# Routed tiles of 256 slots instead of 384, and the gather two tiles ahead, in a recurrence-plus-two-MoE kernel

## The reference: what is computed

```python
noisy_logits = x @ w_gate + np.log1p(np.exp(x @ w_noise)) * noise
top2 = np.argpartition(-noisy_logits, 2, axis=1)[:, :2]
...
for e in range(E):                       # E = 8 experts
    for k in range(2):
        mask = top2[:, k] == e
        h = np.maximum(x[mask] @ w1[e], 0.0)          # 384 -> 1024
        out[mask] += top2_w[mask, k, None] * (h @ w2[e])   # 1024 -> 384
```

## Time and profile before

| | |
|---|---|
| time, 3 runs | median 2584.08 us (2580.21 to 2586.68) |
| span of the profiled execution | 2575.4 us; a time of its own beside the span is not on record |
| PE busy | 2442.9 us (95%) |
| DVE, ACT, POOL busy | 1042.4 (40%), 650.6 (25%), 523.1 us (20%) |
| chain that ended last | PE 73%, DMA 8%, issue 6%, DVE 5%, POOL 5% |
| mean granted TensorE clock | 0.981 |

### The profile page before, as it was taken

One profiled execution on the slowest core, in us unless ns is written; L12 is line 12 of the kernel. 1 busy time (PEld: TensorE's weight loads), 2 busy tenths in 40 slices (PEclk: granted clock), 3 DMA queues, 4 the chain that ended last, 5 costly groups with the idle time before them and its releaser, 6 DMA issues.

```text
span 2575.4 us, 40463 instructions
## 1 busy us (share of the span) xinstructions
PE 2442.9 (95%) x14404; PEld 2422.2 (94%) x14404; DVE 1042.4 (40%) x2039; ACT 650.6 (25%) x1165; POOL 523.1 (20%) x327
## 2 busy tenths in 40 slices
PE   7999999999999999999999999999949999999997
PEld 6989999999999999999999999999849998999897
DVE  8992444333333333333333333334533444343433
ACT  3441111111111111111111111114414444444442
POOL 2112101011011011010110110112343333343333
PEclk9999999999999999999999999999969999999999
DMA  5451000000000000000000000003225555455543
GB/s 134 111 163 64 12 13 24 0 25 24 0 24 18 6 24 0 24 24 0 24 24 0 24 24 0 25 0 62 37 70 158 140 157 174 135 142 141 179 143 62
DMA packets 45907, 155.54 MB, mean 60 GB/s; under 512 B 12992, under 2 KB 32320, under 8 KB 37936
## 3 DMA queue, kind: packets, MB, share of 16 engines
q1 hardware_dynamic: 29984, 127.89, 15.4%
q0 software_dynamic: 15888, 27.19, 5.8%
HBM read 130.23 MB, written 24.82 MB: 60 GB/s over the span
## 4 chain that ended last, share of the span: by engine, by line
PE 73%; DMA 8%; issue 6%; DVE 5%; POOL 5%; ACT 1%; another core or an unknown queue 1%; DVEq 0%; ACTq 0%; POOLq 0%; SPq 0%
PE bank L1082 38%; PE bank L1073 31%; DMA xg<-x,slot_in 4%; DMA out_dram<-ys,slot_out 4%; POOL out_dram L417 3%; POOL xg L428 1%; PE bank L1187 1%; DVE inv L648 1%; DVE decay L642 1%; ACT ys L609 1%; PE bank L991 1%; DVE probs L656 1%; PE bank L1129 1%; DVE state L680 0%
## 5 line engine op out<-in xcount | busy, mean ns | idle before, releaser
L1082 PE MATMUL bank<-w_hi,h_hi 128*128 128x384 f32 x2088 | 712.9, 341 | 4.0 <-DVE h_lo L744 4.0
L1082 PE MATMUL bank<-w_lo,h_hi 128*128 128x384 f32 x2088 | 702.8, 337 | 0.0
L1082 PE MATMUL bank<-w_hi,h_lo 128*128 128x384 f32 x2088 | 702.8, 337 | 0.0
L513 ACT ACTIVATE h_hi<-bank 128x384 fp32r<-128x384 f32 x512 | 251.8, 492 | 1343.0 <-PE bank L1073 1313.4
L1073 PE MATMUL bank<-x_hi,w_hi 128*128 (+1 forms) x1536 | 522.1, 340 | 0.0
L1073 PE MATMUL bank<-x_lo,w_hi 128*128 (+1 forms) x1536 | 520.5, 339 | 0.0
L1073 PE MATMUL bank<-x_hi,w_lo 128*128 (+1 forms) x1536 | 520.4, 339 | 0.0
L744 DVE SCALAR_TENSOR_TENSOR h_lo<-bank,h_hi 128x384 fp32r<-128x384 f32 x512 | 284.9, 557 | 392.2 <-ACT h_hi L513 375.4
L755 DVE SCALAR_TENSOR_TENSOR acc<-bank,route,acc 128x384 f32 (+1 forms) x336 | 186.7, 611 | 589.0 <-PE bank L1082 589.0
L1082 PEld LDWEIGHTS bank<-w_hi,h_hi 128*128 128x128 f32 x2088 | 394.5, 189 | 4.6 <-issue 4.6
L1082 PEld LDWEIGHTS bank<-w_lo,h_hi 128*128 128x128 f32 x2088 | 395.0, 189 | 0.0
(11 more groups left out here) (154 smaller groups left out, 1936.9 us busy)
## 6 DMA issues: line engine op xcount, KB each, us to landing
raw<-wts SPq DMA_DIRECT2D x62, 1536.0 KB, 6.5
qka_sb<-qka SPq DMA_DIRECT2D x48, 288.0 KB, 4.7
out_dram<-zrow SPq DMA_DIRECT2D x1, 5376.0 KB, 17.8
v_sb<-v SPq DMA_DIRECT2D x24, 192.0 KB, 2.5
x<-acc SPq DMA_DIRECT2D x8, 576.0 KB
xg<-x,slot_in POOLq DMA_INDIRECT x69, 5.2
out_dram<-ys,slot_out POOLq DMA_INDIRECT x69
x<-zrow SPq DMA_DIRECT2D x1, 768.0 KB, 18.3
```

The source lines that it names most:

```text
L513: act.activation(h_hi[:, f], ps_h[f][:, 0:TW], ACT.Relu).then_inc(s_hh, 1)
L1082: mm = pe.matmul(ps_o[s][:, 0:DM], hx, w, start=(first and n == 0), stop=(last and n == 2))
```

## The change

Tiles hold RW = 256 slots (RS = 2 slices of 128) instead of 384, and there are (2N - E) // 256 + 8 = 31 of them. Up products move 256 columns, h and the token buffers are taken at that width, down products still move 384 columns but for 2 slices. The plan's arithmetic follows (NS = 12 steps of 256). On POOL the first two tiles are fetched ahead of the loop, and in the loop the fetch of tile t+2 comes ahead of the scatter of tile t. The dense stages keep TW = 384.

```diff
+RW = 256
+RS = RW // P
+NS = N // RW
-SLOTS = RI + TW
+SLOTS = RI + RW
-TILES = (2 * N - E) // TW + E
+TILES = (2 * N - E) // RW + E
...
             def prefetch(tile, p):
-                sp.wait_ge(s_gt, SUB * tile + PRIMED)
+                sp.wait_ge(s_gt, RS * tile + PRIMED)
...
             def scatter(tile, p, pair):
-                pool.wait_ge(s_ys, SUB * (tile + 1) + PRIMED)
+                pool.wait_ge(s_ys, RS * (tile + 1) + PRIMED)
-                for s in range(SUB):
+                for s in range(RS):
...
             split_part(2 * E + 1, 1, 1)
-            with pool.Fori(0, TILES // 2) as pair:
+            fetch(1, 1, 0)
+            with pool.Fori(0, (TILES - 2) // 2) as pair:
                 for p in range(2):
-                    fetch(2 * pair + p + 1, 1 - p, pair + p)
+                    fetch(2 * pair + p + 2, p, pair + 1)
                     scatter(2 * pair + p, p, pair)
-            scatter(TILES - 1, (TILES - 1) % 2, (TILES - 1) // 2)
+            fetch(TILES - 1, (TILES - 1) % 2, (TILES - 1) // 2)
+            for tile in range(TILES - 3, TILES):
+                scatter(tile, tile % 2, tile // 2)
...
             def run_step(tile, p, last):                      # scalar
-                        act.activation(h_hi[:, f], ps_h[f][:, 0:TW], ACT.Relu).then_inc(s_rh, 1)
+                        act.activation(h_hi[:, f, 0:RW], ps_h[f][:, 0:RW], ACT.Relu).then_inc(s_rh, 1)
...
-                for s in range(SUB):
+                for s in range(RS):
                     act.activation(ys[:, p, s], ps_o[s][:, 0:DM], ACT.Copy,
...
             def run_step(tile, p, last):                      # tensor
-                        up(f, *w1, lambda k: xg_hi[:, p, k], lambda k: xg_lo[:, p, k]).then_inc(s_ph, 1)
+                        up(f, *w1, lambda k: xg_hi[:, p, k], lambda k: xg_lo[:, p, k], RW).then_inc(s_ph, 1)
...
-                        down(f, *w2, half == 0 and f == 0, half == 1 and f == FC - 1).then_inc(s_dn, 1)
-                        if half == 1 and not last and f < SUB - 1:
+                        down(f, *w2, half == 0 and f == 0, half == 1 and f == FC - 1, RS).then_inc(s_dn, 1)
+                        if half == 1 and not last and f < RS - 1:
                             turn_gathered(tile + 1, 1 - p, f + 1, (tile + 1) // 2)
```

More of the change, by code:

```diff
@@ L135, in recurrence_and_experts @@
         raw2 = sb("raw2", [P, 2, W1C + W2C])
[L136 to L141, removed]
+        slot_in = sb("slot_in", [P, 2, RS, 2])
+        slot_out = sb("slot_out", [P, 2, RS, 2])
+        xg = sb("xg", [P, 2, RS, DM])
+        xg_hi = sb("xg_hi", [P, 2, KD, RW], FP32R)
+        xg_lo = sb("xg_lo", [P, 2, KD, RW], FP32R)
+        ys = sb("ys", [P, 2, RS, DM])
         bank = [pb(f"bank{i}") for i in range(8)]
@@ L285, in load_slots @@
                 sp.dma_start(buffer[:, p].rearrange("p s w -> p (s w)"),
-                             slots[bass.ds(row, TW)].rearrange("(p s) w -> p (s w)", p=P)).then_inc(loaded[p], 16)
+                             slots[bass.ds(row, RW)].rearrange("(p s) w -> p (s w)", p=P)).then_inc(loaded[p], 16)
             def load_unit(expert, half):
@@ L319, in _ @@
             prefetch(TILES - 2, 1)
-            sp.wait_ge(s_add, 16 * SUB * TILES)
+            sp.wait_ge(s_add, 16 * RS * TILES)
             sp.wait_ge(s_x2, 16 * TS)
@@ L583, in take_tokens @@
             def take_tokens(tile, p):
-                for s in range(SUB):
-                    act.wait_ge(s_gt, SUB * tile + s + 1 + PRIMED)
+                for s in range(RS):
+                    act.wait_ge(s_gt, RS * tile + s + 1 + PRIMED)
                     act.activation(xg_hi[:, p, :, s * P:(s + 1) * P],
@@ L890, in _ @@
             steps.link(dve.tensor_copy(count[:, 0], ps_total))
-            steps.link(dve.tensor_tensor(steps_of[:, 1], count[:, 0].unsqueeze(2).to_broadcast([P, E, E]),
+            steps.link(dve.tensor_tensor(steps_of[:, 1], count[:, 0].unsqueeze(2).to_broadcast([P, E, NS]),
                                          steps_of[:, 0], ALU.is_gt))
@@ L920, in low_tokens @@
             def low_tokens(tile, p):
-                for s in range(SUB):
-                    dve.wait_ge(s_gh, SUB * tile + s + 1)
+                for s in range(RS):
+                    dve.wait_ge(s_gh, RS * tile + s + 1)
                     cols = slice(s * P, (s + 1) * P)
@@ L934, in run_step @@
                         dve.wait_ge(s_rh, n * FC + f + 1)
-                        dve.scalar_tensor_tensor(h_lo[:, f], ps_h[f][:, 0:TW], 0.0, h_hi[:, f].bitcast(FP32),
+                        dve.scalar_tensor_tensor(h_lo[:, f, 0:RW], ps_h[f][:, 0:RW], 0.0, h_hi[:, f, 0:RW].bitcast(FP32),
                                                  ALU.max, ALU.subtract).then_inc(s_rl, 1)
@@ L1072, in up, with down @@
                 for n, (w, x) in enumerate(todo):
-                    mm = pe.matmul(ps_h[f][:, 0:TW], w, x, start=(n == 0), stop=(n == len(todo) - 1))
+                    mm = pe.matmul(ps_h[f][:, 0:width], w, x, start=(n == 0), stop=(n == len(todo) - 1))
                 return mm
-            def down(f, w2h, w2l, first, last):
-                for s in range(SUB):
+            def down(f, w2h, w2l, first, last, subs=SUB):
+                for s in range(subs):
                     rows = slice(s * P, (s + 1) * P)
@@ L1182, in turn_gathered @@
             def turn_gathered(tile, p, s, pair):
-                pe.wait_ge(s_gat[p], 16 * SUB * (pair + 1))
+                pe.wait_ge(s_gat[p], 16 * RS * (pair + 1))
                 if gathered_in(tile, s) is ps_xg:
-                    pe.wait_ge(s_gl, SUB * tile + s + PRIMED)
+                    pe.wait_ge(s_gl, RS * tile + s + PRIMED)
                 for k in range(KD):
@@ L1205, in run_step @@
                     if half == 0:
-                        pe.wait_ge(s_ys, SUB * tile + PRIMED)
+                        pe.wait_ge(s_ys, RS * tile + PRIMED)
                     for f in range(FC):
                         pe.wait_ge(s_rl, n * FC + f + 1)
-                        down(f, *w2, half == 0 and f == 0, half == 1 and f == FC - 1).then_inc(s_dn, 1)
-                        if half == 1 and not last and f < SUB - 1:
+                        down(f, *w2, half == 0 and f == 0, half == 1 and f == FC - 1, RS).then_inc(s_dn, 1)
+                        if half == 1 and not last and f < RS - 1:
                             turn_gathered(tile + 1, 1 - p, f + 1, (tile + 1) // 2)
-            for s in range(SUB):
+            for s in range(RS):
                 turn_gathered(0, 0, s, 0)
```

18 lines of the change are left out of this document (9 added, 9 removed).

## The result

The changed kernel takes 2539.5 us (median of 4 runs, 2538.5 to 2540.0), beside 2582.1 us for the kernel before (2577.2 to 2586.7): ratio 0.9825, 95% interval 0.981 to 0.9839. The prediction was 2580, 2568 to 2606: too slow by 40 us and outside its range. The mechanism that it forecast for a routed tile was there, its length 0.3 us off; what failed above all is what it said of the stage ahead of the tiles.

What follows compares the result with a forecast made beforehand. Before, PE waited for gathers; after, it took the ACT-DVE weight-split chain to bound routed tiles at 20.9 us. The span fell 9.0 us, clock falls added 5, so -4 from 2584.1 gave 2580, range 2568 to 2606.

Steps and rivals of the forecast that it cites:

- The mechanism that it forecast for a routed tile: Routed tile limited by ACT, DVE and PE in turn, since weight splits no longer hide: 20.9 us a tile.
- Half 0 of a tile: Routed tile's first half: downs of chunk 2 wait for h_lo behind DVE's weight pieces; 9.8 us, TensorE alone 8.5.
- The estimate from the 384-column row: Routed up products of 256 columns: stream time plus some 0.013 us each, from 384 columns' price, giving 0.12 us.
- Half 1: Routed tile's second half: slice 1's transposes wait for the bank xg_lo frees, a new gap of about 1.7 us; 11.1 us.
- w_hi starts at 0.56: Half 1 of a routed tile: ACT's w_hi starts 0.56 us after the start of half 0's last down.
- I take four: +5: Routed stage: four clock falls behind the new gap before slice 1, some 1.3 us each, add 5 us.
- The rival with a fall in every second tile: Routed stage: clock falls in every second tile or more, 13 to 20 us instead of 5, 2588 to 2595; chance 0.22.
- The change leaves that stage alone: Dense stage: PE fully busy at full clock, products 0.1745 us apart, taken as not touched by the change.
- The row on which I rested: Dense-stage profile window: 4441 products in 775 us, 0.1745 us apart, used as the price of 384 columns.
- The tail: Behind the last down: ys, scatter and landing, 12.7 us instead of 15.1, with one ys and one scatter less.
- The ring of SP and GpSimd: Rival: scatter, slot_in and gather DMAs set the routed tile, 18.3 to 19 us or more; at 22 us, 2612; chance 0.13.
- It would need DVE's 3.5 us of pieces in a half not to stand ahead of h_lo 2: Condition of the rival that weight splits hide and TensorE alone bounds routed tiles: 93 us less, 2487; chance 0.03.

Runs made afterwards that it cites:

- b_shift: Kernel before with 32 unused bytes a partition ahead of x_hi, so x_hi and x_lo start at a multiple of 64 bytes: 2565.9 us, ratio 0.9947.
- b_addr: Kernel before with 1,632 unused bytes ahead of x_hi, which puts x_hi and x_lo at the changed kernel's addresses: 2567.9 us, ratio 0.9938.
- b_448: Kernel before with 96 unused bytes ahead of x_hi, its address then leaving remainder 448 by 512: 2566.6 us (one run).
- b_512: Kernel before with 160 unused bytes ahead of x_hi, its address then a multiple of 512: 2556.0 us (one run).
- a_dve2: Changed kernel with both VectorE weight pieces behind a half's four h_lo, in half 1 each behind one xg_lo: 2462.3 us, ratio 0.9546.
- a_dve: Changed kernel with VectorE's second weight piece moved behind the last h_lo, in half 1 behind xg_lo too: 2476.5 us, ratio 0.9582.
- b_order: Kernel before (384 slots) with only GpSimd's new order, gather of tile t+2 ahead of scatter of tile t: 2524.6 us, ratio 0.9786.
- bo_addr: Kernel before (384 slots) with GpSimd's new order and 1,632 unused bytes ahead of x_hi: 2511.3 us, ratio 0.9713.
- a_shift: Changed kernel with 32 unused bytes ahead of x_hi, so x_hi and x_lo start 32 bytes past a multiple of 64: 2542.5 us, ratio 0.9853.
- a_old_order: Changed kernel (256 slots) with GpSimd's old order, gather of tile t+1 behind scatter of tile t-1: 2637.7 us, ratio 1.0219.

## Why the prediction was wrong

**Half 0 of a tile: right.** "The last starting 11 x 0.1745 = 1.9 later: 9.8 us" was measured as 9.79 (2198.20 to 2207.99), the products of 256 columns at 0.12 us as 0.120, h_lo at 418 ns against 0.42, h_hi at 388 against 0.38, and the wait stands at chunk 2. The estimate from the 384-column row held. The Trainium skill ("TensorE: Matmul & The Clock Gate", section "Back-to-back issue gap") gives the formula of the prediction, 109 ns for 256 columns, for an isolated product; this trace, where each product has its weight load, does not agree with it (119.6 ns).

**Half 1: 11.1 was 10.77.** "w_hi starts at 0.56" was a wrong reading of the row: 0.55 is the distance from a tile's last down to its ys (2107.13 to 2107.68). In half 1 nothing stands ahead of w_hi, and it starts 0.37 behind the last down, here (2207.99 to 2208.36) as before the change (2119.65 to 2120.02). xg_lo starts at 6.83 instead of 7.05, the transposes at 7.43 instead of 7.76. The tile is 20.57 instead of 20.9, over 29 tiles 9.6 us.

**"I take four: +5" was wrong: no fall.** From the start of the last product ahead of the gap to the start of the first behind it, the gap is 1.75 us (2213.67 to 2215.42). Counted this way the prediction had 2.06 us (7.76 less 5.7); its "1.7 us" is the idle time, which was measured as 1.41. In the five kernels with the old order and 384 slots (before, b_shift, b_addr, b_448, b_512) the 25 falls between the stage's start and its end all stand behind gaps of 2.15 to 2.7 us from start to start. 19 other gaps of 2.15 to 2.6 us had no fall, and of the 61 shorter ones none had. At 1.75 us, and at the 2.06 us of the prediction as well, these traces have no fall; no run lengthened the gap alone. The rival with a fall in every second tile, 0.22, failed with it.

**"The change leaves that stage alone" is the step that failed,** and the largest: the routed stage begins 19.2 us earlier, where the sum had 1.3. The code is the same, but not its operands' addresses, and b_addr shows that these alone give the faster products, some 15 of the 19.2 us. Another 4.0 lie in the last dense unit, whose two lengths no run ties to the change. The row on which I rested, 0.1745 us a product, also mixed prices: 176.6 ns for ups, 174.1 for downs and, as its window runs 46 us into the last unit, the shorter distances of narrow products (700 us by 3994 products are 175.3 ns). I took it for what 384 columns cost. The routed up products of the same shape stood at 173.7; that difference within one trace was there to be asked about.

**The tail** was 11.4 us instead of 12.7. The profiled span was forecast at 2571.4 (2566.4 and 5 for the clock) and came at 2536.4. Of these 35.0 us, 17.9 are the stages ahead (19.2 less the 1.3 that the prediction had for the first gather; some 15 of them by the address), 9.6 the tiles (29 x 0.33), 5 the clock, 1.3 the tail; 1.2 in the first and last tile were not traced. The other 5.6 us are the offset of the median to the span, 8.7 us in the prediction and 3.1 here: that of the kernel before was mostly scatter from run to run, whose times reach from 2577.2 to 2586.7.

**The rivals.** The ring of SP and GpSimd, "18.3 to 19 us", did not bind at 17.99 us (a_dve2), so its sum was too dear; where it binds is open. "It would need DVE's 3.5 us of pieces in a half not to stand ahead of h_lo 2" was the right condition: a_dve (one piece) and a_dve2 (both) make it true, and take 63 and 77 us of the 93 that the prediction had put on it.

**What the change is worth, part by part.** GpSimd's order -55 us at 384 slots. The width, +28 us beside the same order and address, because the two weight pieces that each half must split hid under 12 us of products and no longer hide under 9, in the order in which VectorE does them. The address, some -15 us by the traces (-17.0 from before to b_addr and -13.3 from b_order to bo_addr by the medians), which nobody wrote into the diff.

## What to carry to other kernels

Before taking a stage as untouched, check whether the change moves its buffers: a table that grows by a few hundred bytes shifted all that lay behind it. When a tile is made smaller, list the work per tile that does not shrink and see in what order the helper engine does it: here the order, not the load, cost 2.6 us a tile. And test the parts of a change one by one: one of the two here lost 28 us, looked like a gain only beside the other, and became one when VectorE's work was put in another order.

## What the hardware showed that was not expected

With TensorE busy without a gap at full clock, products of 384 columns started 173.2 to 176.6 ns apart by the SBUF address of the moving operand alone: addresses 150880 and 150912 at 176.6 and 176.1, 150976, 151040, 152512 and 152544 at 173.2, 173.3, 173.2 and 173.7. The routed up products agree (184960 at 176.0; 184800, 184832, 184896 and 186432 at 173.2 to 173.7), and products of 256 columns have such a difference too: 119.6 ns at 183296 (after), 116.7 at 183328 (a_shift), where the tile stayed at 20.6 us as TensorE waits in it. In the profile such a loss is no wait and no idle time; it shows only as fewer products in a stretch that is fully busy.

The clock fell for 3.4 us behind nearly every wait of about 3.2 us for a gather (a_old_order, granted clock 0.92), and behind no gap of the changed kernel (1.00). Near two microseconds the length of the gap does not settle it: from start to start, gaps of up to 2.14 us had no fall in the five kernels with the old order and 384 slots, nor had those of 1.85 to 2.0 us in a_shift, but of the 44 from 2.15 to 2.7 us 25 had one and 19 had none. Between these five kernels the falls differ by number: from first transpose to last down the routed stage took 645.8 us with 2 (b_shift), 651.2 with 3 (b_512), 654.5 with 5 (before), 657.9 with 7 (b_addr) and 659.6 with 8 (b_448). A fall itself is 3.4 us at half clock, at most 1.7 us lost; the rest of the differences is longer gaps (5.3 us more in b_448 than in b_shift) and in b_512 the slower up products (1656 by 2.8 ns, 4.6 us). This also blurs b_addr's and b_448's times beside b_512's.
